# Moving and regrouping the weight loads, maxima and splits beside the attention stage

## The chip, the cores and the metric

The kernel runs on one core of a Trainium2 chip. The metric is device time in microseconds; the median of three runs is given. The core has five instruction streams: TensorE (matmuls and transposes, PE), VectorE (DVE), ScalarE (ACT), GpSimd (POOL) and SyncE (SP, which here only issues DMAs). Each stream runs in order and waits on semaphores.

## The reference

```
attn: q, k, v [4, 8, 576, 64]; scores = q k^T / 8
      heads 0..3: keep 0 <= i - j < 32        (local)
      heads 4..7: keep j <= i, i = j mod 32   (strided)
      softmax, times v  -> x [2304, 512]
moe:  h = x @ w_in [512, 2048];  g = h * sigmoid(1.702 h);  x2 = g @ w_out [2048, 512]
moe2: logits = x2 @ w_gate + log1p(exp(x2 @ w_noise)) * noise;  top 2 of 8 experts, softmax of the two
      out += weight * (relu(x2 @ w1[e]) @ w2[e])        for the two experts e of each token
```

## The kernel before, in words

The kernel has three stages. The first is attention: the 8 heads of 4 batches are taken two at a time, as 16 pairs numbered 0 to 15. Pairs 0 and 1 of each batch are local, 2 and 3 strided. The second stage is the dense feed-forward layer on groups of 256 tokens, the third the routed experts. The change touches the first stage alone.

Every float32 matmul of the feed-forward layers is done as three float16 matmuls. A weight matrix w is scaled by a power of two and split into hi = fp16(w) and lo = fp16(w - hi). The scale needs the largest absolute value of the matrix. So for `w_in` the order is: load raw words into `stage_raw` (L466), take the maximum of each part on VectorE (`w_in_max`, L1076), combine the parts, spread the result over the partitions with one matmul into `ps_all` (L1793, semaphore all_max), reduce it (L1204, semaphore all_read), work out scale and inverse in five dependent tiny instructions (`power_of_two`, L1081 to L1086), then write hi on ScalarE (`weights_hi`, L854) and lo on VectorE (`weights_lo`, L1139). `w_out` is then loaded into the same `stage_raw`, part by part as the lo of `w_in` frees it (L472), and its maxima are taken before attention ends. The first two groups of attention output x get the same treatment: `group_max` (L1115), `group_hi` (L836), `group_lo` (L1111). All this is done beside attention, in slots fixed by hand: the tables `MAX_IN`, `PARTS_IN`, `MAX_OUT`, `HI_X`, `LO_X` say at which pair i each part is taken.

The attention rounds are a software pipeline written out by hand. In round i, TensorE turns q of pair i+2 (L1608 where local, L1616 where strided), finishes p times v of pair i-1 (L1697 local, L1710 strided), turns k of pair i+2, writes masks, turns the probabilities p of pair i (L1677), does the scores of pair i+2 (L1663) and the first half of p times v of pair i. ScalarE evacuates q and k (L810), keeps the finished output (`keep_out`, L831), takes the exponentials of pair i+1 (`exps`, L824) and evacuates p in two pieces (L818), with a `weights_hi` after each piece where one is due. VectorE, in its iteration i, does `weights(i)` (the maxima and splits due there), then `sums(i+1)` (row sums L1104, reciprocal L1107), then `max_and_sub(i+2)` (L1095, L1097). GpSimd multiplies by the reciprocals (`norm`, L653) and TensorE can turn p of a pair only after that.

In iterations 3, 7 and 11 (after pairs 2, 6 and 10) VectorE first waits for `ps_all` and for the output of the pair before to be kept, reduces it and works out the factors, before anything else of the iteration. In the same rounds TensorE waits for all_read before the first half of p times v, because `ps_all` lies in the bank that this writes.

At the end, round 14 runs four pieces of the first feed-forward matmuls ahead (`mlp_ahead`, L1739, 48 matmuls), then spreads the maximum of `w_out` (L1803), which VectorE reduces (L1175), and round 15 closes the stage.

SyncE issues every load of this stage on one queue: q and k of a pair are four DMAs of 144 KB (L458 local, L462 strided), v is 432 KB in three DMAs or 288 KB in two (L395, L399, L405). Before the loop it issues q and k of pairs 0 to 3, v of 0 and 1, the gate weights, and eighths 0, 1 and 2 of `w_in`, 512 KB each. Step i of its loop waits until k of pair i+2 is turned, issues q and k of pair i+4, waits for the turning of p of pair i (p_turned), issues v of pair i+3, waits for the second piece, and issues eighth i+3 of `w_in` or the eighths of `w_out` that `W_OUT_AT` names.

## Time and profile before

| | |
|---|---|
| median of three runs (976.17 to 979.78) | 976.63 us |
| profiled execution, its own time | 979.78 us |
| its span, first to last instruction | 978.1 us |
| PE busy in the span | 930.0 us (95%) |
| DVE busy | 564.3 us (58%) |
| ACT busy | 303.1 us (31%) |
| mean granted TensorE clock | 0.972 |
| chain that ended last, by engine | PE 45%, DVE 33%, ACT 10%, DMA 5% |

The profile is of the slowest of the three runs. Its own time holds 1.7 us outside the span. The granted clock is given as a share of 2.4 GHz: 1.00 is 2.4 GHz, 0.50 is 1.2 GHz. "Idle before" names what ended an idle time of an engine. A duration of an instruction and the step from its start to the next start can differ by some tenths of a microsecond, because neighbours overlap; sums along an engine go by starts.

### The profile page before, as it was taken

How to read it: one execution, taken by the hardware profiler on the slowest of the kernel's cores; microseconds unless marked ns; L12 is line 12 of the kernel's file. 1: busy time of each engine (PE TensorE's matmuls, PEld its weight loads, DVE VectorE, ACT ScalarE, POOL GpSimd, SP SyncE). 2: the span in 40 equal slices, each digit the busy share in tenths (PEclk: the TensorE clock that was granted, in tenths of full speed). 3: DMA queues.
4: the chain of work that ended last, by engine and by line, in shares of the span. 5: the costliest groups of instructions: out<-in, count | busy, mean ns of one | idle time of the engine just before them, and what ended most of it. 6: DMA issues, size and time to landing. Idle time of an engine off the chain costs nothing.

```text
span 978.1 us, 25171 instructions
## 1 busy us (share of the span) xinstructions
PE 930.0 (95%) x10467; PEld 665.2 (68%) x10468; DVE 564.3 (58%) x1030; ACT 303.1 (31%) x412; POOL 198.2 (20%) x269
## 2 busy tenths in 40 slices
PE   8999899999999999999999799899999999999992
PEld 5787686757667675756657576567767777777771
DVE  3469958888888888889986543232332332332231
ACT  4469662423333342334313131111111111111110
POOL 5112200000000000000251332233323333333321
PEclk9689899999999999999999999999999999999997
DMA  9979619675756566575567348565665758474340
GB/s 211 220 172 227 154 40 334 219 264 199 266 187 219 189 215 236 183 256 193 186 225 235 77 114 226 188 189 154 168 185 155 197 131 224 115 222 123 79 87 23
DMA packets 138853, 178.18 MB, mean 182 GB/s; under 512 B 88407, under 2 KB 100695, under 8 KB 136736
## 3 DMA queue, kind: packets, MB, share of 16 engines
q1 hardware_dynamic: 81440, 138.14, 45.2%
q0 software_dynamic: 9600, 27.69, 9.4%
q10 hardware_dynamic: 47744, 11.35, 6.9%
q8 instruction: 53, 0.87, 0.4%
q14 instruction: 16, 0.13, 0.0%
HBM read 112.09 MB, written 53.55 MB: 169 GB/s over the span
## 4 chain that ended last, share of the span: by engine, by line
PE 45%; DVE 33%; ACT 10%; DMA 5%; issue 3%; SPq 1%; POOLq 0%; POOL 0%; ACTq 0%; DVEq 0%
PE bank L1947 19%; PE bank L1956 17%; DVE sc L1076 8%; DVE arena L1265 7%; ACT arena L902 5%; DVE arena L1220 4%; DMA arena<-out,arena 2%; DVE arena L1218 2%; DMA out<-arena 2%; PE bank L1608 2%; PE bank L1847 1%; PE bank L1677 1%; ACT arena L848 1%; DVE x L1111 1%; DVE w_out_s L1139 1%
## 5 line engine op out<-in xcount | busy, mean ns | idle before, releaser
L1739 PE MATMUL bank<-x,w_in_s 128*128 128x256 f16 (+1 forms) x1728 | 195.4, 274 | 0.0
L1847 PE MATMUL bank<-w_out_s,arena 128*128 128x512 f16 x864 | 192.2, 379 | 3.0 <-DVE arena L1220 2.9
L1739 PEld LDWEIGHTS bank<-x,w_in_s 128*128 128x128 f16 x1728 | 169.4, 98 | 23.9
L1847 PEld LDWEIGHTS bank<-w_out_s,arena 128*128 128x128 f16 x864 | 82.7, 98 | 100.0 <-DVE arena L1220 6.4
L1538 DVE TENSOR_TENSOR arena<-arena 128x512 f32<-128x512 f32 x37 | 25.6, 692 | 168.6 <-ACT arena L999 92.8
L1947 PEld LDWEIGHTS bank<-arena,w_out_s 128*128 128x128 f16 x2016 | 114.5, 98 | 5.8 <-issue 0.7
L1947 PE MATMUL bank<-arena,w_out_s 128*128 128x128 f16 x2016 | 116.9, 219 | 0.6 <-issue 0.6
L1947 PEld LDWEIGHTS bank<-arena,w_in_s 128*128 128x128 f16 x1920 | 109.1, 98 | 6.7 <-issue 2.2
L1947 PE MATMUL bank<-arena,w_in_s 128*128 128x128 f16 x1920 | 111.6, 219 | 1.5 <-DMA arena<-arena 1.4
L1956 PE MATMUL bank<-w_out_s,arena 128*128 128x512 f16 x480 | 108.6, 383 | 4.4 <-DVE arena L1533 4.4
L1956 PE MATMUL bank<-w_in_s,arena 128*128 128x512 f16 x480 | 106.9, 379 | 2.3 <-DVE arena L1533 2.3
L1076 DVE TENSOR_REDUCE sc<-arena 128x1 f32<-128x512 f32 (+2 forms) x50 | 102.2, 2045 | 3.7 <-ACT arena L908 3.4
L1531 DVE CAST arena<-arena 128x512 f16<-128x512 f32 x82 | 35.3, 431 | 116.7 <-ACT arena L994 102.6
L994 ACT ACTIVATE arena<-bank 128x512 f32<-128x512 f32 x82 | 49.0, 597 | 169.6 <-PE bank L1947 150.7
L1265 DVE SCALAR_TENSOR_TENSOR arena<-arena,sc 128x4096 f16<-128x4096 f32 x16 | 71.7, 4482 | 26.4 <-ACT arena L902 26.4
L1956 PEld LDWEIGHTS bank<-w_out_s,arena 128*128 128x128 f16 x480 | 46.5, 99 | 57.7 <-issue 6.9
L902 ACT ACTIVATE arena<-arena,sc 128x4096 f16<-128x4096 f32 x16 | 59.3, 3709 | 82.9 <-DVE sc L1086 82.9
L999 ACT ACTIVATE arena<-bank,arena 128x512 f32<-128x512 f32 x40 | 27.5, 687 | 183.6 <-PE bank L1956 180.4
L1956 PEld LDWEIGHTS bank<-w_in_s,arena 128*128 128x128 f16 x480 | 46.1, 98 | 54.5 <-DVE arena L1533 2.1
L717 POOL DMA_INDIRECT arena<-out,arena x37 | 43.5, 1177 | 131.8 <-DMA out<-arena 116.6
L722 POOL DMA_INDIRECT out<-arena x40 | 41.7, 1043 | 107.1 <-DVE arena L1538 101.4
L1533 DVE TENSOR_TENSOR arena<-arena 128x512 f16<-128x512 f32 x82 | 56.8, 693 | 2.8
(219 smaller groups left out, 830.8 us busy)
## 6 DMA issues: line engine op xcount, KB each, us to landing
arena<-in_moe_w SPq DMA_DIRECT2D x16, 2048.0 KB, 9.7
split_weights<-arena SPq DMA_DIRECT2D x16, 2048.0 KB, 7.4
w_in_s<-split_weights SPq DMA_DIRECT2D x32, 512.0 KB
w_out_s<-split_weights SPq DMA_DIRECT2D x32, 512.0 KB
arena<-in_q SPq DMA_DIRECT2D x32, 144.0 KB, 3.2
arena<-in_k SPq DMA_DIRECT2D x32, 144.0 KB, 3.9
out<-zeros SPq DMA_DIRECT2D x1, 4608.0 KB, 21.5
x_rows<-arena SPq DMA_DIRECT2D x18, 256.0 KB, 2.2
```

Of the source, the lines that this page charges most:

```text
L717: pool.indirect_dma_start(out=prior[b4 % 2], out_offset=None, in_=out, in_offset=bass.IndirectOffsetOnAxis(ap=cur[b4], axis=0), bounds_che ...
L722: pool.indirect_dma_start(out=out, out_offset=bass.IndirectOffsetOnAxis(ap=cur[b4], axis=0), in_=ysb[b4 % 2], in_offset=None, bounds_check ...
L902: nc.scalar.activation(halves[:, 0], raw[m], ACT.Copy, scale=col(S_U + m)).then_inc(S["unit_hi"], 1)
L994: nc.scalar.activation(hf[half], ps_dh[half], ACT.Relu, scale=DOWN).then_inc(S["relu_done"], 1)
L1076: return nc.vector.tensor_reduce(dst, src, AX.X, ALU.max, apply_absolute_value=True)
L1220: nc.vector.scalar_tensor_tensor(lo, gf[fq % 2], of_group(G_X, t), hi, ALU.mult, ALU.subtract).then_inc(S["g_lo"], 1)
L1265: nc.vector.scalar_tensor_tensor(halves[:, 1], raw[m], col(S_U + m), halves[:, 0], ALU.mult, ALU.subtract).then_inc(S["unit_lo"], 1)
L1533: V.tensor_tensor(lo, hf[half], hi, ALU.subtract).then_inc(S["h_lo"], 1)
L1739: last = mm(dst, w_in_s[:, w_part, c, f * P:(f + 1) * P], group_half(x_part, t)[:, c], start=(c == 0 and w_part + x_part == 0), stop=(c == ...
L1847: last = mm(ps_x[j], g[par][:, g_part, f, j * P:(j + 1) * P], w_out_s[:, w_part, f], start=(n == 0), stop=(n == 3 * FC - 1))
L1947: last = mm(ps_dh[half][:, n * P:(n + 1) * P], w1_of(w_par, w_part, c, f), xt[par][:, x_part * DC + c], start=(c == 0 and w_part + x_part ...
L1956: last = mm(ps_y[par], h[par][:, h_part, f * P:(f + 1) * P], w2_of(w_par, w_part, f), start=(n == 0), stop=(n == 3 * EFC - 1))
```

## The change

Loads and maxima of `w_in` and loads of `w_out` go from eight parts of 512 KB to four quarters of 1 MB. Before the loop only quarter 0 of `w_in` is loaded, where eighths 0, 1 and 2 were; quarters 1, 2 and 3 follow in the loop steps of pairs 4, 5 and 7 (`W_IN_AT`, i = 2, 3, 5 in the new numbering, which is two ahead of the old). The quarters of `w_out` go out in the loop steps of pairs 13 and 14 and twice after the loop. The loop's waits for p_turned are gone. The splits are still done by eighths. The tables of iterations change: maxima of `w_in` in iterations 2 to 5, group maxima both in 8, hi of `w_in` in rounds 8 to 12 instead of 7 to 11 and lo one later, maxima of `w_out` in 12 to 14 instead of 9 and 12 to 14, hi of group 1 in round 13 instead of 14, lo of group 1 in iteration 14 instead of 15. In iterations 3, 7 and 11 VectorE now does the weights and the row sums first, then reduces `ps_all`, then does `max_and_sub`, and works out the factors last.

```diff
--- before.py
+++ after.py
@@ -67,14 +67,12 @@
 
 QUARTERS = 4
 BUSY = 16
-SPLIT_OUT = 15
+MAX_IN, SPLIT_OUT = 2, 15
 LAST_IN, LAST_X, LAST_OUT = 6, 10, 14
-MAX_X = 7
-MAX_IN = {2: (0, 1), 3: (2,), 4: (3, 4), 5: (5, 6), 6: (7,)}
-PARTS_IN = {7: (0,), 8: (1, 2), 9: (3, 4), 10: (5, 6), 11: (7,)}
-HI_X, LO_X = {12: 0, 14: 1}, {13: 0, 15: 1}
-MAX_OUT = {9: (0,), 12: (1, 2), 13: (3, 4), 14: (5, 6, 7)}
-assert max(MAX_IN) <= LAST_IN < min(PARTS_IN)
+MAX_X = 8
+PARTS_IN = {8: (0, 1), 9: (2, 3), 10: (4,), 11: (5, 6), 12: (7,)}
+MAX_OUT = {12: (0, 1), 13: (2, 3, 4), 14: (5, 6, 7)}
+assert MAX_IN + QUARTERS <= LAST_IN < min(PARTS_IN) - 1
 CONSTS = 12 + 2 + 1 + 4 + 1 + SQ // SRES + 2
 
 FULL = (2 * TOK) // P
@@ -300,7 +298,7 @@
 
 
         S = {n: sem(n) for n in (
-            "consts_pool busy_set qk_in0 qk_in1 v_in0 v_in1 v_in2 v_in3 w_raw0 w_raw1 w_raw2 w_raw3 w_raw4 w_raw5 w_raw6 w_raw7 "
+            "consts_pool busy_set qk_in0 qk_in1 v_in0 v_in1 v_in2 v_in3 w_raw0 w_raw1 w_raw2 w_raw3 "
             "small_in noise_in t_done t_evac s_done mx_done sub_done exp_done sum_done rr_done norm_done pv_done "
             "o_kept x_hi x_lo x_max x_all x_step x_scaled raw_max scaled step split_hi split_lo "
             "raw_in0 raw_in1 unit_max unit_all unit_scaled unit_hi unit_lo unit_out "
@@ -312,7 +310,7 @@
             "held turning out_zero zero_done prior_in0 prior_in1 y_sum y_out w_even w_odd xg_zero"
         ).split()}
         qk_in = [S["qk_in0"], S["qk_in1"]]
-        w_raw = [S[f"w_raw{i}"] for i in range(2 * QUARTERS)]
+        w_raw = [S[f"w_raw{i}"] for i in range(QUARTERS)]
         v_in = [S[f"v_in{i}"] for i in range(4)]
         raw_in = [S["raw_in0"], S["raw_in1"]]
         x2_store = [S["x2_store0"], S["x2_store1"]]
@@ -447,6 +445,8 @@
 
         @block.sync
         def _(sp):
+            w_in_raw = stage_raw.rearrange("p (c f) -> p c f", c=DC)
+            w_out_raw = stage_raw.rearrange("p (c n) -> p c n", c=FC)
 
             def load_qk(b, hp):
                 par = hp % 2
@@ -463,19 +463,19 @@
                                          ).then_inc(qk_in[par], 16)
 
             def load_w_in(n):
-                sp.dma_start(eighth_raw(n), w_in.rearrange("(c p) (a f) -> p c a f", p=P, a=2)[:, n // 2, n % 2]
+                c = DC // QUARTERS
+                sp.dma_start(w_in_raw[:, n * c:(n + 1) * c], w_in.rearrange("(c p) f -> p c f", p=P)[:, n * c:(n + 1) * c]
                              ).then_inc(w_raw[n], 16)
 
             def load_w_out(n):
-                c = FC // QUARTERS // 2
-                sp.wait_ge(S["split_lo"], n + 1)
-                sp.dma_start(eighth_raw(n).rearrange("p (c n) -> p c n", c=c),
+                c = FC // QUARTERS
+                sp.wait_ge(S["split_lo"], 2 * n + 2)
+                sp.dma_start(w_out_raw[:, n * c:(n + 1) * c],
                              w_out.rearrange("(c p) n -> p c n", p=P)[:, n * c:(n + 1) * c]).then_inc(w_raw[n], 16)
 
             load_qk(0, 0)
             load_qk(0, 1)
             load_w_in(0)
-            load_w_in(1)
             sp.wait_ge(S["t_done"], 4)
             load_qk(0, 2)
             load_v(sp, 0, 0)
@@ -484,27 +484,25 @@
             load_v(sp, 0, 1)
             sp.dma_start(wg[:, :, 0:E], w_gate.rearrange("(c p) e -> p c e", p=P)).then_inc(S["small_in"], 16)
             sp.dma_start(wg[:, :, E:16], w_noise.rearrange("(c p) e -> p c e", p=P)).then_inc(S["small_in"], 16)
-            load_w_in(2)
-
-            W_OUT_AT = {8: (0,), 9: (1, 2), 10: (3, 4), 11: (5, 6)}
-            for i in range(NPAIR - PAIRS):
-                q_turned, p_turned = 8 * i + 12, 8 * i + 14
-                sp.wait_ge(S["t_done"], q_turned)
-                load_qk((i + 4) // PAIRS, (i + 4) % PAIRS)
-                if i == 0:
+
+            W_IN_AT, W_OUT_AT = {2: 1, 3: 2, 5: 3}, {11: 0, 12: 1}
+            for i in range(2, NPAIR - 2):
+
+                sp.wait_ge(S["t_done"], 8 * i - 4)
+                load_qk((i + 2) // PAIRS, (i + 2) % PAIRS)
+                if i == 2:
                     load_v(sp, 0, 2)
-                sp.wait_ge(S["t_done"], p_turned)
-                if i > 0:
-                    sp.wait_ge(S["pv_done"], i)
-                load_v(sp, (i + 3) // PAIRS, (i + 3) % PAIRS)
-                sp.wait_ge(S["t_done"], p_turned + 2)
-                if i + 3 < 2 * QUARTERS:
-                    load_w_in(i + 3)
-                for n in W_OUT_AT.get(i, ()):
-                    load_w_out(n)
+                else:
+                    sp.wait_ge(S["pv_done"], i - 2)
+                load_v(sp, (i + 1) // PAIRS, (i + 1) % PAIRS)
+                if i in W_IN_AT:
+                    load_w_in(W_IN_AT[i])
+                if i in W_OUT_AT:
+                    load_w_out(W_OUT_AT[i])
             sp.wait_ge(S["pv_done"], NPAIR - PAIRS)
             load_v(sp, BATCH - 1, PAIRS - 1)
-            load_w_out(2 * QUARTERS - 1)
+            load_w_out(2)
+            load_w_out(3)
 
             sp.dma_start(noise_sb[:], noise.rearrange("(t p) e -> p t e", p=P)).then_inc(S["noise_in"], 16)
 
@@ -873,8 +871,8 @@
                     exps(i + 1)
                 evac_pt(p_use, hp, 0)
                 parts = PARTS_IN.get(i, ())
-                if HI_X.get(i) == 0:
-                    group_hi(0)
+                if i in (LAST_X + 2, LAST_X + 3):
+                    group_hi(i - LAST_X - 2)
                 elif parts:
                     weights_hi(parts[0], w_in_s, S_WI, 1)
                     parts = parts[1:]
@@ -885,7 +883,6 @@
                     weights_hi(n, w_in_s, S_WI, 1)
                 if i == NPAIR - 2:
                     exps(i + 1)
-                    group_hi(1)
                 if i == NPAIR - 1:
                     act.wait_ge(S["scaled"], 3)
                     gelu(0, 0)
@@ -1121,13 +1118,13 @@
             def w_in_max(n):
 
                 dve.wait_ge(w_raw[n], 16)
-                step(absmax(col(PART_MAX + n), eighth_raw(n)))
-                if n == 2 * QUARTERS - 1:
-                    absmax(col(B_MAX), col(PART_MAX, 2 * QUARTERS)).then_inc(S["raw_max"], 1)
+                step(absmax(col(PART_MAX + n), quarter_raw(n)))
+                if n == QUARTERS - 1:
+                    absmax(col(B_MAX), col(PART_MAX, QUARTERS)).then_inc(S["raw_max"], 1)
 
             def w_out_max(n):
 
-                dve.wait_ge(w_raw[n], 32)
+                dve.wait_ge(w_raw[n // 2], 32)
                 step(absmax(col(PART_MAX + n), eighth_raw(n)))
                 if n == 2 * QUARTERS - 1:
                     absmax(col(B_MAX), col(PART_MAX, 2 * QUARTERS)).then_inc(S["raw_max"], 1)
@@ -1157,19 +1154,19 @@
                     dve.wait_ge(S["small_in"], 32)
                     nc.vector.tensor_reduce(col(B_MAX), wg[:], AX.XY, ALU.max, apply_absolute_value=True
                                             ).then_inc(S["raw_max"], 1)
-                for n in MAX_IN.get(i, ()):
-                    w_in_max(n)
-                if i in (MAX_X, MAX_X + 1):
+                if MAX_IN <= i < MAX_IN + QUARTERS:
+                    w_in_max(i - MAX_IN)
+                if i == MAX_X:
                     dve.wait_ge(S["o_kept"], PAIRS + 1)
-                    step(group_max(PART_MAX + i - MAX_X, i - MAX_X))
-                if i == MAX_X + 1:
+                    step(group_max(PART_MAX, 0))
+                    step(group_max(PART_MAX + 1, 1))
                     absmax(col(B_MAX), col(PART_MAX, 2)).then_inc(S["raw_max"], 1)
                 for n in PARTS_IN.get(i - 1, ()):
                     weights_lo(n, w_in_s, S_WI, 0)
                 for n in MAX_OUT.get(i, ()):
                     w_out_max(n)
-                if i in LO_X:
-                    group_lo(LO_X[i])
+                if i in (LAST_X + 3, LAST_X + 4):
+                    group_lo(i - LAST_X - 3)
                 if i == NPAIR - 1:
                     dve.wait_ge(S["all_max"], 4)
                     nc.vector.tensor_reduce(col(WO_ALL), ps_all_out, AX.X, ALU.max).then_inc(S["out_max"], 1)
@@ -1198,17 +1195,18 @@
                 w_out_lo(i)
 
             for i in range(NPAIR):
+                weights(i)
+                if i + 1 < NPAIR:
+                    sums(i + 1)
                 if i - 1 in ALL_OF:
                     dve.wait_ge(S["all_max"], i // PAIRS + 1)
                     dve.wait_ge(S["o_kept"], i + 1)
                     nc.vector.tensor_reduce(col(ALL_OF[i - 1]), ps_all, AX.X, ALU.max).then_inc(S["all_read"], 1)
+                if i + 2 < NPAIR:
+                    max_and_sub(i + 2)
+                if i - 1 in ALL_OF:
                     dve.wait_ge(S["all_read"], i // PAIRS + 1)
                     weights_factors(i - 1)
-                weights(i)
-                if i + 1 < NPAIR:
-                    sums(i + 1)
-                if i + 2 < NPAIR:
-                    max_and_sub(i + 2)
             weights_factors(NPAIR - 1)
 
             def split_g(t, par, fq):
```

## Rows read from the trace of the kernel before

**Rows 1.** Stretches of the span: engine busy us (instructions), PEclk, DMA share, GB/s.

```profile
0.00:128.70 128.70, 115.62 (x2740) 92.39 (x2741) 85.82 (x115) 74.25 (x165) 35.72 (x64) 0.85 0.80 187
...
29.61:56.92 27.31, 27.31 (x539) 23.03 (x534) 14.00 (x17) 12.42 (x29) 3.71 (x3) 0.50 0.90 203
...
63.40:69.60 6.20, 6.16 (x206) 5.16 (x205) 3.79 (x7) 3.85 (x10) 1.28 (x2) 1.00 0.81 181
```

**Rows 2.** Waits of TensorE, 0 to 135 us: total us, times, longest.

```profile
PE bank L1677 <- POOL arena L653: 4.7, 4, 1.9
```

**Rows 3.** TensorE in time: start, us, line, [idle before]: rounds 1 to 3, round 5.

```profile
26.99 0.69 PE L1697 MATMUL bank<-arena 96*64 96x64 f32 x16
...
29.30 0.19 PE L1623 MATMUL bank<-busy_in 128*128 128x28 bf16 x1 [1.63 <-DMA arena<-in_k]
...
39.75 1.53 PE L1608 MATMUL bank<-ident,arena 48*64 48x48 f32 x48
...
57.81 0.71 PE L1616 MATMUL bank<-ident,arena 96*128 96x96 f32 x6
```

**Rows 4.** SyncE in time: the load of eighth 2 of w_in.

```profile
20.30 0.51 SPq L466 DMA_DIRECT2D arena<-in_moe_w_in  x1
```

**Rows 5.** DMAs by line, k of pair 4, then pair 5: first and last start, landing.

```profile
L458 SPq DMA_DIRECT2D arena<-in_k x2: 432/818/1204, 21.8 to 23.1; - x2
...
DMA to landing us min/median/max: 4.4/4.8/6.1
...
L458 SPq DMA_DIRECT2D arena<-in_k x2: 433/1043/1653, 26.7 to 28.4; - x2
...
DMA to landing us min/median/max: 7.1/7.7/8.2
```

**Rows 6.** Round 7 in time: ScalarE, VectorE (up to iteration 8), TensorE.

```profile
72.99 1.01 ACT L824 ACTIVATE arena<-arena 128x960 f32<-128x960 f32 x1
...
72.07 0.29 DVE L1204 TENSOR_REDUCE sc<-bank 128x1 f32<-128x128 f32 x1 [1.36 <-ACT x L831]
...
73.53 1.22 DVE L1115 TENSOR_REDUCE sc<-x 128x1 f32<-128x1024 f32 x1
...
80.82 1.15 DVE L1104 TENSOR_REDUCE arena<-arena 128x10 f32<-128x960 f32 x1
...
75.12 0.67 PE L1710 MATMUL bank<-arena 36*64 36x36 f32 x32
```

**Rows 7.** Rounds 11 to 14 in time: ScalarE exps(12), then VectorE.

```profile
97.40 1.01 ACT L824 ACTIVATE arena<-arena 128x960 f32<-128x960 f32 x1
...
96.47 0.29 DVE L1204 TENSOR_REDUCE sc<-bank 128x1 f32<-128x128 f32 x1 [0.95 <-ACT x L831]
...
98.29 2.47 DVE L1139 SCALAR_TENSOR_TENSOR w_in_s<-arena,sc,w_in_s 128x1024 f16<-128x1024 f32 x2
...
100.68 1.15 DVE L1104 TENSOR_REDUCE arena<-arena 128x10 f32<-128x960 f32 x1
...
101.99 1.10 DVE L1095 TENSOR_REDUCE arena<-bank 128x10 f32<-128x960 f32 x1
...
104.20 1.27 DVE L1139 SCALAR_TENSOR_TENSOR w_in_s<-arena,sc,w_in_s 128x1024 f16<-128x1024 f32 x1
...
105.39 2.47 DVE L1076 TENSOR_REDUCE sc<-arena 128x1 f32<-128x1024 f32 x2
...
107.89 1.16 DVE L1104 TENSOR_REDUCE arena<-arena 128x10 f32<-128x960 f32 x1
...
110.62 2.46 DVE L1076 TENSOR_REDUCE sc<-arena 128x1 f32<-128x1024 f32 x2
...
113.12 1.28 DVE L1111 SCALAR_TENSOR_TENSOR x<-x,sc 128x1024 f16<-128x1024 f32 x1
...
114.32 0.75 DVE L1104 TENSOR_REDUCE arena<-arena 128x16 f32<-128x576 f32 x1
...
116.67 3.72 DVE L1076 TENSOR_REDUCE sc<-arena 128x1 f32<-128x1024 f32 x3
```


## The prediction

> **What bounds the kernel now.** I read the table of stretches first. The change touches only attention and what runs beside it, and that stage ends at about 128.7 us [rows 1]. What follows has the same instructions before and after, in the same order, and starts from what the stage leaves; so I carry a shift of the stage's end to the end of the kernel one to one. In the stage VectorE is busy 85.8 of 128.7 us and TensorE's mean granted clock is 0.85 [rows 1]; neither alone says what binds, so I read it in time, stretch by stretch.
>
> First stretch, to about 57 us: transfers and the clock. TensorE ends the first half of p times v of pair 1 at 27.7 and stands still until q and k of pair 4 are there; its next matmul is at 29.30, and the row names in_k for 1.63 us of idle time [rows 3]. The last k DMA of that pair is issued at 23.1 and lands 6.1 us later, at 29.2 [rows 5]. Right behind this idle time the granted clock is 0.50 (1.2 GHz) for 27.3 us, with the DMA engines busy 90% of it at 203 GB/s [rows 1]. Rounds 3 and 4 run in that stretch and take 57.81 - 39.75 = 18.1 us [rows 3], where a round at 1.00 takes 6.2 us [rows 1]. Next stretch, from 63 us: rounds of 5.7 to 6.5 us, passed between TensorE, ScalarE and VectorE. Last stretch, rounds 11 to 15: VectorE. It works nearly without a gap from 96.47 on [rows 7], and what TensorE waits for is the normalized p: 4.7 us in four waits [rows 2], each behind VectorE's row sums.
>
> The terms are worked out against the profiled execution, 979.78 us (span 978.1 and 1.7 around it). It is the slowest of three; the median is 3.15 us lower. I add the change to the median, since nothing here makes it depend on what differs between these runs, except the length of the slow-clock stretch, which stays in the range.
>
> **The early loads.** Eighth 2 of w_in, 512 KB, is issued at 20.30 [rows 4], just ahead of q and k of pair 4 on the same queue. The change takes it from there. At the 203 GB/s of that stretch 512 KB are 2.6 us, so k of pair 4 lands at 29.2 - 2.6 = 26.6 instead, before the 27.7 at which TensorE asks. The wait of 1.63 us goes. What is late next: by the time of q and k of pair 5, both versions have put the same bytes into the queue (2 MB of w_in, the same q, k and v), because quarter 1 now goes out in the first loop step. That k lands at 28.4 + 8.2 = 36.6 before [rows 5], behind a queue that never ran dry, and I keep 36.6 for after. Before, TensorE asked for it only at 39.75, since round 2 ran at the slow clock. Now round 2 can start at 27.7 at the full clock, is done 6.2 us later at 33.9, and TensorE stands still for 2.7 us until 36.6. That is longer than the idle time that preceded the fall before, so I expect the clock to fall there, and rounds 3 and 4 to run slowly as they did. Gain: 39.75 - 36.6 = 3.2 us at the start of round 3. Least: if the clock falls at 29.6 all the same, round 2 runs as before, 1.6 us early, and 1.6 us stay; none stays if larger loads ahead of pair 6 make that one late. Most: full clock throughout; then each round is bounded by its transfers. To the start of round 5, three rounds of 6.2 us from 27.7 plus 2.7 of waiting end at 49.0, plus 2.6 for the extra 512 KB that then lie ahead of pair 6: 51.6 against 57.81, 6.2 us. I take 3.2, range 0 to 6.2.
>
> The Trainium skill (TensorE: Matmul & The Clock Gate, Terms) prices time at the low clock at that time times one minus the granted share. By that the 27.3 us cost 13.7 us, and keeping the clock would give 13.7 instead of 6.2. The rows say less, since part of those rounds waits for transfers anyhow.
>
> The dropped waits for p_turned on SyncE let v and w_in go out one or two microseconds sooner, behind q and k of the same step; nothing on TensorE waits for v in these rows. I cost it at nothing, and at up to 1 us if a megabyte lies in front of q and k of pair 6; that is inside the bound of 0. The maxima of w_in cost VectorE the same words in four instructions as in eight, saving four fixed starts of under 0.1 us each beside idle time: nothing. Quarter 3 must be there in iteration 5; it is issued with round 3's k and has a round and a half.
>
> **Iterations 7 to 9.** Before, VectorE waits 1.36 us for the kept output and reduces ps_all at 72.07 [rows 6]. After, the row sums of pair 8 come first. They need exps(8), which end at 72.99 + 1.01 = 74.0. Then 74.0 + 1.31 (row sums and reciprocal of a local pair, 100.68 to 101.99 [rows 7]) + 0.33 (the reduce) = 75.6, when TensorE may start p times v of pair 7, which it starts at 75.12 before: 0.5 us late. The hi part that leaves ScalarE in this round gives up to 1.0 us, but it is behind this wait and is lost. VectorE goes on: + 2.21 (max_and_sub, local, 101.99 to 104.20) + 1.15 (factors) + 2.5 (both group maxima, one of them 1.22 [rows 6]) = 81.5 for the row sums of pair 9, against 80.82: 0.7 us late, of the same delay. I take +0.6 us, bounds -1.0 (ScalarE's gain comes through) and +1.0. In iterations 9 and 10 VectorE has less to do than before, but the rounds are then passed on by ScalarE, still with two hi parts in rounds 8 and 9, and by TensorE: its free time is not turned into anything.
>
> **Iterations 11 to 14, the main loss.** With that 0.6, exps(12) end at 98.4 + 0.6 = 99.0 [rows 7]. VectorE is free by about 96.7 and idles until then. From there it is the bound, and its work up to the row sums of pair 14 is, by steps from start to start [rows 7]: row sums 12, 1.31; reduce and factors, 1.82 (96.47 to 98.29); max_and_sub 13, 2.21; lo of eighths 5 and 6, 2.39 (98.29 to 100.68); maxima 0 and 1 of w_out, 2.50 (105.39 to 107.89); row sums 13 and max_and_sub 14, 2.73 (107.89 to 110.62); lo of 7, 1.19 (104.20 to 105.39); three maxima, 3.72; lo of group 0, 1.20 (113.12 to 114.32). Sum 19.1, so 99.0 + 19.1 = 118.1 against 114.32: 3.8 us late. Before, the same span held one maximum less and did one lo and one maximum in the light iterations 8 and 9. The norm of pair 14, TensorE's turning of it, and the four pieces of mlp_ahead follow it directly, so the stage ends 3.8 us later, this time the 0.6 included. The three maxima of iteration 14 and the lo of group 1, now ahead of row sums 15, lie beside mlp_ahead, which covers them: they end at about 127, it at 132. Without that cover they would cost 1.2 us.
>
> Gains inside: the wait of 1.55 us at round 12 for norm(12) goes, since the row sums of pair 12 start at 99.0 and not at 100.68; it returns in round 13 and 14 as a longer one. Bounds of this term: 2.0 (the light rounds 9 to 11 run 1.8 us faster than I allow) and 5.5 (mlp_ahead, which runs at 0.50 for most of its time before, meets a longer slow stretch, 1.7 us more).
>
> **Sum.** -3.2 + 3.8 = +0.6 us: 980.4 for the profiled execution, 977.2 for the median.
>
> **Rivals.**
> A, forecast: early gain of about 3, late loss of about 4, 976 to 979.
> B, the clock falls as before. For it: rounds with the small transposes leave little work per microsecond even when TensorE is occupied. Gain 1.6, loss 3.8: +2.2, 978.8.
> C, full clock through rounds 2 to 4. For it: the wait that preceded the fall is gone. Against: transfers still bind and TensorE must stand still before round 3 and 4. -6.2 + 3.8 = -2.4, 974.2; with the late loss at its lower bound 2.0, 972.4, and with ScalarE's 1.0 as well, 971.4.
> D, slower: the pile on VectorE. Row sums of pairs 13 and 14 come behind 4.9 and 6.1 us of weight work in iterations 12 and 13 instead of 3.7 and 3.7. It decides from the point where the early gain is under 1 us: either the clock falls at 29.6, or 1 MB ahead of pair 6 starves round 4 and the slow clock lasts into round 6. Then 0 + 5.5 = +5.5: 982.1.
> E, the loads don't matter and the early stretch is unchanged because another transfer (v, or the slowest of the DMA engines) holds k of pair 4 up to 29: 0 + 3.8, 980.4; it is B with nothing gained.
>
> **Chances.** A 0.40, B and E 0.22, C 0.15, D 0.23. A measurement here tells a change from none at about 0.5%, 4.9 us: faster means under 971.7, slower over 981.5. Under 971.7 lies the far end of C and some of what I have not seen: 0.09. Over 981.5 lie D, mostly, and a little of E: 0.26. The rest, 0.65, is the same. A's own range is 975 to 979; the range for 8 in 10 goes from 971.5 (C at its bounds) to 983.5 (D with another microsecond of waiting).
>
> **What would show it.** Right: no idle time of TensorE named in_k near 28 us, but one of 2 to 3 us near 34 to 36; the clock 1.00 in round 2, then 0.50; round 3 starting near 36.6 and round 5 near 54.6; TensorE's wait for norm(12) gone and those for norm(13) and norm(14) longer, 3 us or more each; VectorE without a gap from the row sums of pair 12 on; L1175 near 129 (128.4 before, +0.6). Wrong: the clock at 1.00 through to round 5 (C), or 0.50 past 60 us (D); row sums of pair 14 less than 2 us after or more than 6 us after those before, measured from the end of exps(12); or a shift of the stages behind 128.7 us that isn't that of the stage's end.

## The result and the profile after

The changed kernel takes 983.98 us, the median of seven runs (982.05 to 989.32), against 978.11 for the kernel before in seven runs beside it (976.08 to 981.26). The ratio is 1.007, with a 95% interval of 1.004 to 1.010: slower, by about 5.9 us, where 977.2 and a range of 971.5 to 983.5 were forecast. The forecast started from 976.63, the median of three runs; the kernel before is at 978.11 in the seven. So 1.5 us of the miss of 6.8 lie in that, and 5.3 in the change itself: +5.9 measured for +0.6 forecast.

The profiled execution of the changed kernel is its fastest, and not one of the seven: 979.09 us, span 977.4. That is less than the 979.78 of the profiled execution before, so the two totals say nothing; the stages have to be read one by one. The end of the attention stage is where VectorE reduces the last `ps_all`: L1175 before, L1172 after. That row starts at 128.38 before and 133.99 after, 5.6 us later. How near this is to the 5.9 us between the medians is partly luck: a second profile of the changed kernel has the row at 136.10. The row before:

```profile
128.38 0.29 DVE L1175 TENSOR_REDUCE sc<-bank 128x1 f32<-128x128 f32 x1 [5.74 <-PE bank L1803]
```

**Behind the stage.** From there to about 610 us the same matmul of the second and third stages starts 5.6 us later in the trace after, wherever one compares: matmul number 2800 from the start at 132.77 and 138.38, number 5100 at 448.76 and 454.36, number 6500 at 604.83 and 610.45. What turns the totals round is one event in the kernel before that the trace after lacks. First a row of TensorE there (start, length, idle time ahead of it), then the piece of the chain of waits that leads to it:

```profile
623.00 3.52 PE L1956 MATMUL bank<-w_out_s,arena 128*128 128x512 f16 x9 [4.40 <-DVE arena L1533]
...
611.70 8.95 DMA arena<-out,arena
```

A DMA of 9 us leaves TensorE idle for 4.4 us, and a stretch at the low clock follows; together about 6.2 us. Such an event (a DMA of 6.9 to 9.7 us between 605 and 634 us, and 2.9 to 5.5 us of idle TensorE behind it) shows in 6 of the 14 profiles of this study, of kernels of both kinds. In the other eight the work behind the stage takes 843 to 846 us, in these six 847 to 854. So in these traces a shift of the stage does carry on one to one, and a total of one execution can't be read against another. How often the event falls into the timed runs of each kernel is not known, since only profiled executions show it.

**The early loads.** The wait for k of pair 4 [rows 3] is gone. Its last DMA is issued at 21.6 and takes at most 4.3 us, so it is there by 26 us, where [rows 5] have it at 29.2:

```profile
L458 SPq DMA_DIRECT2D arena<-in_k x2: 431/436/441, 21.1 to 21.6; - x2
...
DMA to landing us min/median/max: 3.0/3.0/4.3
```

TensorE goes into round 2 at 28.54 without a wait, at full clock, which it keeps until 32.2. And it gets hardly further than before. TensorE in time, after (start, length, line, idle time ahead):

```profile
28.65 0.91 PE L1606 MATMUL bank<-ident,arena 48*64 48x48 f32 x48
29.50 0.42 PE L1695 MATMUL bank<-arena 96*64 96x32 f32 x7
33.18 1.22 PE L1695 MATMUL bank<-arena 96*64 96x32 f32 x17 [3.26 <-issue]
...
40.70 0.92 PE L1606 MATMUL bank<-ident,arena 48*64 48x48 f32 x48
...
42.53 0.49 PE L1606 MATMUL bank<-ident,arena 48*64 48x48 f32 x17
44.31 0.68 PE L1606 MATMUL bank<-ident,arena 48*64 48x48 f32 x31 [1.29 <-issue]
...
54.48 0.68 PE L1695 MATMUL bank<-arena 96*64 96x64 f32 x14
56.36 0.33 PE L1695 MATMUL bank<-arena 96*64 96x64 f32 x2 [1.20 <-issue]
57.12 0.71 PE L1614 MATMUL bank<-ident,arena 96*128 96x96 f32 x6 [0.42 <-issue]
```

TensorE stops three times in the middle of a run of like matmuls, after 7 of 24, after 17 of 48 and after 14 of 16, and each time for nothing that the profile shows ("issue"). These stops and the short one at 57.12 are 6.2 us in sum. Round 3 starts at 40.70 (39.75 before), round 5 at 57.12 (57.81). Of the two queues in the DMA view of 28 to 35 us, one carries instructions, the other the loads:

```profile
q1 hardware_dynamic: 1871, 1.61, 107.9%
q8 instruction: 2, 0.03, 2.5%
...
arena<-in_moe_w_in SPq DMA_DIRECT2D x1, 1024.0 KB, 10.3
```

In 28 to 35 us 16-KB packets of instructions go through the same DMA engines as a 1-MB load that takes 10.3 us to land. One of them is under way from 30.5 to 31.8, and TensorE resumes at 33.18; others end at 42.8 and 54.8, and TensorE resumes at 44.31 and 56.36. Every profile but that of the kernel before has such stops, 40 in all: each comes after 594, 718, 843 or 1092 matmuls of the trace, and each ends 1.0 to 1.7 us after a packet of that queue has ended. (In 9 of them a further stop of 0.3 to 0.4 us, as the one at 57.12, comes two matmuls after the last.) So what TensorE lacks there are its own instructions.

**The late part.** VectorE, rounds 11 to 15, and the end of the stage; it answers to [rows 7], where the row sums of pairs 12, 13 and 14 stand at 100.68, 107.89 and 114.32:

```profile
91.81 0.75 DVE L1101 TENSOR_REDUCE arena<-arena 128x16 f32<-128x576 f32 x1 [0.41 <-ACT arena L822]
...
98.50 1.15 DVE L1101 TENSOR_REDUCE arena<-arena 128x10 f32<-128x960 f32 x1 [2.23 <-ACT arena L822]
...
104.06 2.48 DVE L1136 SCALAR_TENSOR_TENSOR w_in_s<-arena,sc,w_in_s 128x1024 f16<-128x1024 f32 x2
106.45 2.47 DVE L1073 TENSOR_REDUCE sc<-arena 128x1 f32<-128x1024 f32 x2
108.95 1.15 DVE L1101 TENSOR_REDUCE arena<-arena 128x10 f32<-128x960 f32 x1
...
111.68 1.63 DVE L1136 SCALAR_TENSOR_TENSOR w_in_s<-arena,sc,w_in_s 128x1024 f16<-128x1024 f32 x1
113.23 3.71 DVE L1073 TENSOR_REDUCE sc<-arena 128x1 f32<-128x1024 f32 x3
116.98 1.28 DVE L1108 SCALAR_TENSOR_TENSOR x<-x,sc 128x1024 f16<-128x1024 f32 x1
118.18 0.74 DVE L1101 TENSOR_REDUCE arena<-arena 128x16 f32<-128x576 f32 x1
...
133.99 0.29 DVE L1172 TENSOR_REDUCE sc<-bank 128x1 f32<-128x128 f32 x1 [7.39 <-PE bank L1801]
```

From the row sums of pair 11 to those of pair 14 it is 26.37 us, where the same took 22.04 before: 4.3 us more. The row sums of pair 11 before:

```profile
92.28 0.75 DVE L1104 TENSOR_REDUCE arena<-arena 128x16 f32<-128x576 f32 x1
```

Ahead of the row sums of pair 14 lie 6.5 us of splits and maxima (111.68 to 118.18), the pile of what follows. Then ScalarE and TensorE in the same rounds, after:

```profile
112.85 0.76 ACT L816 ACTIVATE arena<-bank 96x384 f32<-96x384 f32 x2 [0.38 <-PE bank L1675]
118.37 1.15 ACT L834 ACTIVATE x<-x,sc 128x1024 f16<-128x1024 f32 x1 [4.75 <-DVE x L1108]
119.42 0.74 ACT L816 ACTIVATE arena<-bank 96x384 f32<-96x384 f32 x2
```

```profile
114.38 0.69 PE L1695 MATMUL bank<-arena 96*64 96x64 f32 x16
119.94 1.55 PE L1695 MATMUL bank<-arena 96*64 96x32 f32 x24 [4.88 <-ACT arena L816]
121.42 2.28 PE L1675 MATMUL bank<-ident,arena 128*128 128x128 f32 x8
```

The hi part of group 1 (L834), moved to round 13, waits 4.75 us on ScalarE for the lo part of group 0 (L1108), which VectorE does behind its three maxima. Behind L834 in ScalarE's order is the second copy of the turned p(13) (L816), and for that TensorE idles 4.88 us. In this stretch, 111.1 to 121.4, TensorE is busy 4.24 of 10.30 us at a mean granted clock of 0.81; it is at 1.2 GHz from 117.6 to 131.2:

```profile
111.10:121.40 10.30, 4.24 (x115) 3.66 (x115) 10.13 (x11) 3.24 (x6) 2.28 (x2) 0.81 0.47 111
```

### The profile page after: what moved, and what is told of

The parts are those of the page before. It is cut to its first block, busy times and chain, and to the rows that moved or that the text cites. A ratio compares the mean times of both kernels' runs of the same rounds, so it can differ in the third digit from the quotient of the medians.

```text
span 977.4 us, 25136 instructions
## 1 busy us (share of the span) xinstructions
PE 925.3 (95%) x10467; PEld 661.2 (68%) x10468; DVE 564.0 (58%) x1026; ACT 302.6 (31%) x412; POOL 196.4 (20%) x269
## 4 chain that ended last, share of the span: by engine, by line
PE 48%; DVE 34%; ACT 9%; issue 4%; DMA 2%; POOL 0%; ACTq 0%; POOLq 0%; SPq 0%; DVEq 0%
PE bank L1945 20%; PE bank L1954 19%; DVE sc L1073 8%; DVE arena L1263 7%; ACT arena L899 5%; DVE arena L1218 4%; DVE arena L1216 2%; PE bank L1675 2%; PE bank L1606 1%; PE bank L1845 1%; PE bank L1661 1%; ACT arena L846 1%; DVE x L1108 1%; DVE w_out_s L1136 1%; PE bank L1695 1%
## 5 line engine op out<-in xcount | busy, mean ns | idle before, releaser
L1073 DVE TENSOR_REDUCE sc<-arena 128x1 f32<-128x512 f32 (+3 forms) x46 | 101.6, 2209 | 3.6 <-ACT arena L905 3.4
```

The lines of the kernel that those rows point to most:

```text
L1073: return nc.vector.tensor_reduce(dst, src, AX.X, ALU.max, apply_absolute_value=True)
```

## The experiments

Each ran beside the kernel before on the same chip. To read the cause I use three stretches of the first stage in each one's profiled execution: to the row sums of pair 5, from there to those of pair 11, and from there to the end of the stage. The ratio comes from all timed runs of both kernels and can differ by 0.2% from the ratio of the two medians; "stops" is the sum of TensorE's idle time put down to "issue" between 16 and 64 us.

```
                        to p.5  5 to 11  11 to 14  11 to end  end     stops  ratio [95%]
before                   54.68   37.60    22.04     36.10    128.38   0.0
after                    53.48   38.33    26.37     42.18    133.99   6.2    1.007  [1.004, 1.010]
change, once more        55.90   38.03    26.37     42.17    136.10   7.7    1.010  [1.006, 1.014]
group 1 back             54.83   38.02    26.03     40.14    132.99   4.9    1.007  [1.003, 1.011]
factors first            53.74   46.57    25.38     40.55    140.86   9.4    1.005  [1.002, 1.009]
eighth loads back        50.64   37.15    26.03     40.47    128.26   3.2    1.001  [0.998, 1.004]
w_in later               48.62   38.25    27.04     42.34    129.21   1.5    0.998  [0.995, 1.002]
three maxima left out    54.19   45.72    22.28     38.02    137.93   11.3   1.000  [0.998, 1.003]
late part spread         53.72   39.97    24.13     37.57    131.26   7.6    1.000  [0.997, 1.003]
quarter loads only       53.26   38.94    22.01     36.96    129.16   6.9    0.999  [0.996, 1.003]
quarter loads, again     54.99   37.27    22.03     33.62    125.88   5.6    1.000  [0.997, 1.004]
before, loads later      48.82   39.46    22.03     33.62    121.90   3.7    1.000  [0.997, 1.003]
before, later, again     48.84   38.70    22.04     35.97    123.51   4.0    1.001  [0.997, 1.004]
spread and later         47.20   43.41    23.72     37.26    127.87   2.7    1.002  [0.999, 1.004]
```

The stretches are of one execution each, and three kernels were profiled twice. From pair 11 to 14 the two profiles of a kernel agree within 0.02 us, to the end they do not: 36.96 and 33.62, 33.62 and 35.97, though 42.18 and 42.17 for the change. The piece behind the row sums of pair 14 goes with the granted clock: 11.6 us at 0.92, 13.4 to 14.4 at 0.63 to 0.76, 15.0 to 15.8 at 0.59 to 0.67. And the profiled execution is the fastest of its kernel in after, the change once more, eighth loads back and the first of loads later, the slowest in factors first, three maxima left out, and spread and later. So the end of the stage in one row can't be held against the ratio beside it.

**Group 1 back.** Of the changed kernel, hi of group 1 goes back to round 14 and lo to iteration 15.

```diff
-                if i in (LAST_X + 2, LAST_X + 3):
-                    group_hi(i - LAST_X - 2)
+                if i == LAST_X + 2:
+                    group_hi(0)
...
                 if i == NPAIR - 2:
                     exps(i + 1)
+                    group_hi(1)
...
-                if i in (LAST_X + 3, LAST_X + 4):
-                    group_lo(i - LAST_X - 3)
+                if i in (LAST_X + 3, LAST_X + 5):
+                    group_lo((i - LAST_X - 3) // 2)
```

> The changed kernel with hi and lo of group 1 put back where they were before (round 14 and iteration 15). Theory P (pile on VectorE, and beside it a wait of ScalarE): in the changed kernel ScalarE stands 4.75 us in round 13, because hi of group 1 waits for lo of group 0, and the second piece of p of pair 13 lies behind it; TensorE stands 4.88 us. Without it that piece goes out near 115, but the row sums of pair 14 still start near 118, so p of pair 14 is turned near 120.5 instead of 121.4, and the stage ends 1 to 3 us earlier (L1172 near 131 to 133 instead of 134.0): 981 to 983 for the median. Rival W (the wait of ScalarE is the whole loss): L1172 near 129, median 978 to 979. Rival E (the early loads are the loss): no difference to the changed kernel, 984.

Measured: 985.82 us (980.62 to 994.88), 1.007; the expected 981 to 983 were missed. In the trace the idle time of 4.88 us is gone and TensorE waits 2.21 us for the normalized p instead:

```profile
116.59 2.40 PE L1696 MATMUL bank<-arena 96*64 96x64 f32 x40
121.20 2.28 PE L1676 MATMUL bank<-ident,arena 128*128 128x128 f32 x8 [2.21 <-POOL arena L651]
```

From pair 11 to the end it is 2.0 us less than after: 0.3 up to the row sums of pair 14, 0.9 from there to the turning of its p (2.32 us for 3.24), and 0.8 behind it, where the clock was higher. The wait of L834 is real, but at most 0.9 us can be put down to it, and not safely: with three maxima left out (below) it is 1.0 us long, and TensorE, then at 1.2 GHz, takes up p of pair 14 3.23 us behind the row sums all the same. It is not the main cause: the row sums of pair 14 stay late, and the median does not fall.

**Eighth loads back.** The changed kernel with the loads and maxima of `w_in` by eighths, and the loop of SyncE with its waits for p_turned, as before; the rest is the change's.

```diff
-MAX_IN, SPLIT_OUT = 2, 15
+SPLIT_OUT = 15
+MAX_IN = {2: (0, 1), 3: (2,), 4: (3, 4), 5: (5, 6), 6: (7,)}
...
+                sp.wait_ge(S["t_done"], p_turned + 2)
+                if i + 3 < 2 * QUARTERS:
+                    load_w_in(i + 3)
```

> The changed kernel with w_in loaded and its maxima taken by eighths at the places of before, and the loop waits of SyncE as before; all the rest of the change stays. Theory P: TensorE's three stops inside a run of matmuls (3.26, 1.29 and 1.20 us, waiting for nothing that the profile shows) go, the wait for k of pair 4 and the slow clock from 30 to 57 us come back, round 5 starts near 57.8; the late part is as in the changed kernel, row sums of pair 14 near 119, end near 134.5; median 983 to 985. Rival E: the early loads are the loss: median near 978.

Measured: 980.62 us, 1.001; 983 to 985 were expected, with the clock low from 30 to 57 us and round 5 near 57.8, and all three were missed. The wait for k is back, 1.90 us; the stops for "issue" are 3.2 us, about half of those after; pair 5 comes at 50.64. The pile stays (26.03). So with the pile in place, the old loads are worth about 5 us by the medians: 1.0 us over the kernel before beside it, where the change is 5.9 over.

**Quarter loads only**, run twice: the kernel before with `w_in` in four loads of 1 MB at the change's steps.

```diff
-MAX_IN = {2: (0, 1), 3: (2,), 4: (3, 4), 5: (5, 6), 6: (7,)}
+MAX_IN = {2: (0,), 3: (1,), 4: (2,), 5: (3,)}
...
+            W_IN_AT = {0: 1, 1: 2, 3: 3}
...
-                if i + 3 < 2 * QUARTERS:
-                    load_w_in(i + 3)
+                if i in W_IN_AT:
+                    load_w_in(W_IN_AT[i])
```

> The kernel before with the early part alone: w_in loaded in four quarters of 1 MB at the steps of the change, maxima in iterations 2 to 5; everything else as before. Theory P: k of pair 4 is there in time, TensorE stops inside matmul runs appear as in the changed kernel, round 5 starts at 57 +- 1, row sums of pair 14 near 113.5 to 114.5, L1175 near 128; median within 1.5 us of before, 977 to 979. Rival E: median 983 or more.

> The kernel of e3 (before, with the early part of the change alone) in five rounds. If the early part of the change neither gains nor loses, because the wait for k has only become stops for instructions: within 1.5 us of before. If the megabyte loads cost in themselves: 2 to 4 us over before. If my forecast of the early part was right after all: 3 us under before.

Measured: 977.26 and 973.89 us, 0.999 and 1.000. The medians are 2.3 us under those of the kernel before beside them both times, but the ratio over all runs is within 0.1% of 1, and its interval reaches 0.36% to either side. Alone, the large loads neither gain the forecast 3 us nor cost anything that can be told from the spread, though TensorE's stops are 6.9 and 5.6 us in sum.

**Factors first.** The changed kernel with the old order in iterations 3, 7 and 11: the reduction of `ps_all` and the factors ahead of the row sums.

```diff
             for i in range(NPAIR):
-                weights(i)
-                if i + 1 < NPAIR:
-                    sums(i + 1)
                 if i - 1 in ALL_OF:
...
+                    dve.wait_ge(S["all_read"], i // PAIRS + 1)
+                    weights_factors(i - 1)
+                weights(i)
+                if i + 1 < NPAIR:
+                    sums(i + 1)
```

> The changed kernel with the reduction of the spread maximum and the factors put back to the front of iterations 3, 7 and 11. Theory P: iteration 11 again waits for the kept output and does 1.8 us of factors before lo of eighth 4 and the row sums of pair 12, which start near 99.5 to 100 instead of 98.5; the work after it is the same less 1.8, so row sums of pair 14 come near 117.5 to 118.2, as in the changed kernel or up to 0.7 us earlier; median 983 to 984.5. Rival O (the new order is what costs): 980 or less.

Measured: 984.00 us, 1.005, not told from the change. So the order of the factors shows no part in the loss.

**w_in later.** The changed kernel with quarters 1 to 3 loaded from round 5 on. The four maxima of `w_in` are then all taken of quarter 0, so its factor is another number.

```diff
-            W_IN_AT, W_OUT_AT = {2: 1, 3: 2, 5: 3}, {11: 0, 12: 1}
+            W_IN_AT, W_OUT_AT = {7: 1, 8: 2, 9: 3}, {11: 0, 12: 1}
...
+                if scaled == 1 and n % 2 == 0:
+                    act.wait_ge(w_raw[n // 2], 16)
...
-                dve.wait_ge(w_raw[n], 16)
-                step(absmax(col(PART_MAX + n), quarter_raw(n)))
+                dve.wait_ge(w_raw[0], 16)
+                step(absmax(col(PART_MAX + n), quarter_raw(0)))
```

> The changed kernel with quarters 1 to 3 of w_in loaded from round 5 on instead of rounds 0 to 3, so that 3 MB fewer compete in the first 50 us; the maximum is taken four times of quarter 0 (this part of the computation is changed). Theory F (instructions of TensorE come late because the DMA engines are full): the stops inside runs of matmuls (3.3, 1.3, 1.2 us in the changed kernel) shrink to under 0.5 us in all, there is no wait for k, the clock stays at 1.00 past 35 us, round 5 starts at 47 to 51 instead of 57, and the median is 5 to 9 us under the changed kernel: 975 to 979. Rival G (they come late by themselves, whatever the traffic): the stops stay at 4 us or more in all and the median is within 2 us of 984.

Measured: 976.13 us (971.09 to 979.44), 0.998. TensorE's rows, the same stretch as the rows of the early loads above:

```profile
29.03 0.42 PE L1697 MATMUL bank<-arena 96*64 96x32 f32 x7
29.60 0.74 PE L1697 MATMUL bank<-arena 96*64 96x32 f32 x17 [0.15 <-issue]
...
34.11 0.32 PE L1710 MATMUL bank<-arena 36*64 36x36 f32 x7
34.63 0.59 PE L1710 MATMUL bank<-arena 36*64 36x36 f32 x25 [0.20 <-issue]
...
37.11 0.69 PE L1608 MATMUL bank<-ident,arena 48*64 48x48 f32 x17
38.94 1.10 PE L1608 MATMUL bank<-ident,arena 48*64 48x48 f32 x31 [1.14 <-issue]
...
50.53 0.71 PE L1616 MATMUL bank<-ident,arena 96*128 96x96 f32 x6 [0.23 <-ACT arena L816]
```

The stop after 7 of 24 falls from 3.26 to 0.15 us, and round 5 starts at 50.53 instead of 57.12. The DMA engines move less; the stretch 20 to 50 us, after and here:

```profile
20.00:50.00 30.00, 25.02 (x643) 20.51 (x643) 16.17 (x20) 15.10 (x37) 5.90 (x4) 0.83 0.90 213
```

```profile
20.00:50.00 30.00, 27.73 (x772) 22.68 (x771) 20.28 (x24) 18.29 (x45) 5.90 (x4) 0.89 0.74 168
```

So with 3 MB moved away the stops shrink from 6.2 to 1.5 us, where under 0.5 was expected. Between the first two stops 124 matmuls run and between the next two 125, each with a weight load of its own: about 250 instructions, in every kernel at the same places of the code.

The amount of traffic alone doesn't order the profiles, though. In the same 30 us the five with `w_in` by eighths move 217 to 226 GB/s and stop for 0.0 to 4.0 us in sum; the eight with 1-MB loads at the change's steps move 200 to 218 GB/s and stop for 4.9 to 11.3. Spread and later has the most traffic of all:

```profile
20.00:50.00 30.00, 26.29 (x763) 21.39 (x750) 18.52 (x26) 17.89 (x45) 7.22 (x5) 0.94 0.98 226
```

That points at the size of a load that lies ahead; but the steps at which the loads go out differ too, and no run changes the size alone.

**Three maxima left out.** The changed kernel without the maxima of eighths 2 to 4 of `w_out`; its factor comes from eighths 5 to 7 alone.

```diff
-MAX_OUT = {12: (0, 1), 13: (2, 3, 4), 14: (5, 6, 7)}
+MAX_OUT = {12: (0, 1), 14: (5, 6, 7)}
```

> The changed kernel without the three maxima of w_out in iteration 13 (left out of the computation, with those of iteration 12 out of the combination). Theory P (pile on VectorE): lo of group 0 and the row sums of pair 14 come 3.7 us earlier, near 114.5, ScalarE's wait in round 13 falls from 4.75 to about 1 us, the stage ends 3.5 to 5 us earlier (L1172 near 129 to 130.5); median 979 to 981. Rival W2 (the loss is in the order of the waits, the pile has slack): less than 1.5 us earlier.

Measured: 979.43 us, 1.000. Pair 11 to pair 14 falls from 26.37 to 22.28 us, and ScalarE's wait with it to 1.0 us. VectorE, iterations 13 and 14:

```profile
119.44 1.63 DVE L1136 SCALAR_TENSOR_TENSOR w_in_s<-arena,sc,w_in_s 128x1024 f16<-128x1024 f32 x1
120.99 1.27 DVE L1108 SCALAR_TENSOR_TENSOR x<-x,sc 128x1024 f16<-128x1024 f32 x1
122.19 0.74 DVE L1101 TENSOR_REDUCE arena<-arena 128x16 f32<-128x576 f32 x1
```

3.7 us of VectorE work taken away from one place give back 4.1 us there and 4.2 us by the time of the stage's end (38.02 for 42.18). The profiled execution ends its stage late all the same, at 137.93 where 129 to 130.5 was expected, since its early stops happened to be 11.3 us and its clock low from 60 to 70 us; it is the slowest of its ten, and the median does not show that.

**Late part spread.** Nothing left out: the changed kernel with group 1 back, the group maxima in iterations 7 and 8, and the maxima of `w_out` from iteration 11.

```diff
-MAX_X = 8
+MAX_X = 7
-MAX_OUT = {12: (0, 1), 13: (2, 3, 4), 14: (5, 6, 7)}
+MAX_OUT = {11: (0, 1), 12: (2,), 13: (3, 4), 14: (5, 6, 7)}
...
```

> The changed kernel with group 1 back in round 14 and iteration 15, the group maxima one each in iterations 7 and 8, and the maxima of w_out 0 and 1 in iteration 11 (where VectorE idles 2.2 us), 2 in 12, 3 and 4 in 13. Theory P: VectorE's work between the exponentials of pair 12 and the row sums of pair 14 falls by 2.5 us, these come near 115.7, and the stage's end (L1173) is 3.5 to 5 us earlier than the changed kernel's 134.0; median 979 to 981. Rival: under 1.5 us.

Measured: 977.99 us, 1.000. From pair 11 to pair 14 it is 24.13 us instead of 26.37, the 2.2 us that were forecast as 2.5; to the end 37.57 instead of 42.18.

**Before, loads later**, run twice: the kernel before with eighths 2 to 6 of `w_in` loaded one or two loop steps later, so that none but 0 and 1 goes out ahead of the loop.

```diff
-            load_w_in(2)
+            W_IN_AT = {1: (2,), 2: (3,), 3: (4, 5), 4: (6, 7)}
-MAX_IN = {2: (0, 1), 3: (2,), 4: (3, 4), 5: (5, 6), 6: (7,)}
+MAX_IN = {2: (0, 1), 4: (2,), 5: (3, 4), 6: (5, 6, 7)}
...
```

> The kernel before with the eighths of w_in later: none in loop step 0, eighth 2 in step 1, 3 in step 2, 4 and 5 in step 3, 6 and 7 in step 4, maxima 2; 3, 4; 5, 6, 7 in iterations 4, 5, 6. 1 MB fewer lies ahead of q and k of pairs 4 to 7. Theory F: no wait for k of pair 4, shorter stops, round 5 starts at 51 to 54 instead of 57.8; two heavy iterations cost 1 to 2 us; median 2 to 5 us under before. Rival G: within 1.5 us of before.

> The kernel of e7 (before, with the eighths of w_in later) in five rounds, for the question whether it beats before. Theory F: 2 to 5 us under before; its stops of TensorE under 4 us in all. Rival G: within 1.5 us of before.

Measured: 977.05 and 977.46 us, 1.000 and 1.001. No wait for k, stops of 3.7 and 4.0 us, pair 5 at 48.8 in both. Yet the ratio does not move, and the expected 2 to 5 us under the kernel before were missed both times. In the two traces the stage ends 5 to 6.5 us before that of the kernel before; that this shows in no ratio is not explained.

**Spread and later**: both edits on the changed kernel, the late part spread and the loads by eighths, later.

> The changed kernel with both repairs: the late part spread as in e8 (group 1 back, group maxima in 7 and 8, maxima of w_out 0, 1 in iteration 11, 2 in 12, 3 and 4 in 13) and w_in by eighths at the later steps of e7. If late pile and early traffic are the two causes and add: 4 us from the first, 3 to 5 from the second against the changed kernel, so 975 to 977, 1 to 3 us under before. If only the late pile counts: 978 to 980.

Measured: 977.97 us, 1.002; the expected 975 to 977 were missed. Pair 5 comes at 47.20, the earliest of all, but the next stretch is 43.41 us, with a low clock from 66 to 79.7 us. **The change, once more**, to have its size twice:

> The changed kernel once more, unchanged, beside the three that follow, to size the loss on one chip and to see the early stops a second time. From the row sums of pair 11 to those of pair 14: 26.4 +- 0.5 us as in its first profile (22.0 before); the early stops of TensorE 5 us or more in all; median 5 to 7 us over before.

Measured: 986.59 us (980.70 to 987.46, six runs), 1.010, 10.5 us over the kernel before where 5 to 7 were expected, and the wait of 4.88 us on TensorE again. No version here beats the kernel before.

## Why the prediction was wrong

**Late part: right in place, too small, and its one good figure is luck.** The row sums of pair 14 were forecast at 118.1 and started at 118.18. But the 118.1 leaves out the early gain; with the 3.2 us of the sum it would be 114.9. Counted from the row sums of pair 5, which lie ahead of all that the late part moves, the row sums of pair 14 come 64.70 us behind, for 59.64 before: 5.1 us more, where 3.8 were forecast. Of that, 0.7 us lie before pair 11 (0.6 forecast), exps(12) came about 0.5 us later after pair 11, and pair 12 to pair 14 took 19.68 us, 3.8 more than from the end of exps(12) before, for 19.1 and 3.2 forecast. TensorE's wait at round 12 for the normalized p is gone, and those at rounds 13 and 14 are longer, as forecast (2.45 us, and the 4.88 us that hides the other). The rows for pair 5, before and after:

```profile
54.68 1.15 DVE L1104 TENSOR_REDUCE arena<-arena 128x10 f32<-128x960 f32 x1 [2.10 <-ACT arena L824]
```

```profile
53.48 1.15 DVE L1101 TENSOR_REDUCE arena<-arena 128x10 f32<-128x960 f32 x1 [0.68 <-ACT arena L822]
```

Taking three maxima out of the pile, or spreading it, brings the ratio from 1.007 and 1.010 to 1.000. But so do the two runs that keep the pile and change when and how `w_in` is loaded (1.001 and 0.998, with 26.03 and 27.04 us from pair 11 to pair 14). So as far as the ratios go the pile is needed for the loss, and so are the large early loads; neither is its cause alone.

**The end of the stage: one wait was missed.** "The norm of pair 14, TensorE's turning of it, and the four pieces of mlp_ahead follow it directly, so the stage ends 3.8 us later." I moved hi of group 1 to round 13 without asking for what it waits: lo of group 0, which I had put behind the maxima in the very same sum, and p(13) is queued behind it on ScalarE. TensorE so takes up p(14) at 121.42 instead of 116.64 (4.8 us later, where the row sums are 3.9 later) and runs the rest at the low clock: the 48 matmuls of mlp_ahead take 8.01 us for 7.59. From the row sums of pair 14 to the end it is 15.8 us for 14.1, 1.7 us more, 0.9 of it at p(14) and the rest behind it. After, then before:

```profile
125.89 8.01 PE L1737 MATMUL bank<-x,w_in_s 128*128 128x256 f16 x48
```

```profile
116.64 0.66 PE L1677 MATMUL bank<-ident,arena 128*128 128x128 f32 x4 [1.94 <-POOL arena L653]
...
120.70 7.59 PE L1739 MATMUL bank<-x,w_in_s 128*128 128x256 f16 x48
```

How much of the 1.7 us is the wait and how much the clock isn't separated: this piece took 15.7 us also where the wait was only 1.0 us (three maxima left out), and 14.1 with group 1 back.

**Early loads: the failed step.** "Now round 2 can start at 27.7 at the full clock, is done 6.2 us later at 33.9 ... Gain: 39.75 - 36.6 = 3.2 us at the start of round 3." Round 2 did start at 28.54 at the full clock. But TensorE then ran dry of instructions, for 6.2 us in sum, which no row of the kernel before had as a wait. There, all of rounds 2 to 4 ran at 1.2 GHz [rows 1], the packets of instructions came too, and TensorE never stopped for one; that the slower pace hid them is my reading. Round 3 started 0.95 us later than before instead of 3.2 earlier, and round 5 0.7 us earlier instead of 3.2. The idle time of 2 to 3 us for k of pair 5 that I named did not show; k was there. In all eight profiles with loads by quarters at the change's steps pair 5 comes at 53.3 to 55.9 us, the 54.68 of before in their midst. At the row sums of pair 5 the gain is 1.2 us in this trace, and in the ratios of quarter loads only (0.999 and 1.000) it is nothing that can be told. At rounds 3 and 5 this is rival D's condition, an early gain under 1 us, by a mechanism that I had not named. Its price of 5.5 us lies near the 5.9 measured by luck: it had 1.7 us for a longer slow stretch in mlp_ahead, which took 0.4 us more, and it had nothing for the missed wait. The four starts of maxima that I priced at under 0.1 us each were 0.6 us in sum (2.28 us for a quarter, 1.21 for an eighth); they lie beside idle time all the same.

The Trainium skill (Runtime: NRT & Kernel Launch, Instruction fetch mechanics) says that an engine's instructions are fetched through a DMA queue of its own in blocks of 16 KiB, or 256 instructions, and that this is mostly hidden. The 16-KB packets and the stops some 250 instructions apart agree with the first; that it is hidden does not hold here, with up to 5.5 us in one stop. The Trainium skill (DMA: Bandwidth & Descriptors, Queues, rings and completion order) has each DMA engine take turns between queues packet by packet; no run here shows the turns themselves.

**Iterations 7 to 9** were right in size: forecast 0.6 us later; the row sums of pair 8 start 1.5 us earlier than before and those of pair 9 0.3 later, and from pair 5 to pair 11 it is 0.7 us more (38.33 for 37.60). The second profile of the change has 0.4.

**The sum, by the traces.** To the row sums of pair 5 -1.2 us, where -3.2 were forecast at round 3; from there to the end of the stage +0.7 and +6.1, where 3.8 were forecast for both. Together +5.6. So the early term is off by 2.0 us and the late one by 3.0, both to the same side. The carry was right: behind the stage these two traces stay 5.6 us apart up to 610 us.

**What stays open.** The two halves don't add up. Large loads cost nothing that shows on the kernel before (0.999, 1.000), and neither does the late pile with the loads by eighths (1.001); only together are they 0.7 to 1.0% slower. In the profiles one sees half of it: with the old loads in the changed kernel pair 5 comes at 50.64, 2.6 to 5.3 us ahead of the quarters, which pays for the pile. But then the kernel before should gain as much over its version with quarters, and it does not. The waits for p_turned were put back only together with the eighth loads, so their part isn't separated either. Nor is it shown what makes the instruction packets late: the run that moved loads away changed the amount of traffic, the rates over all profiles speak for the size of a load, and the steps were never held fixed. And the event of 6 us behind the stage may fall into the timed runs of one kernel more often than into those of another; no run rules that out as a part of the 0.7%.

Where the low clock falls varies too. It was 0.50 for 27 us in the one profile of before; with the same loads in the changed kernel it was not.

## What to carry to other kernels

When an instruction is moved, write down what it waits for in its new place and what is queued behind it on its engine; a wait of 4.75 us came here from a part that was itself moved at no cost. A wait that is taken away where the DMA engines are 90% busy can come back under another name, here 1.63 us for k as 6.2 us for instructions. So ask what the next transfer, be it the engine's own instructions, allows. And sum the work of the busiest engine between two events on the path: that gave 19.1 us here for 19.7 measured.

## What the hardware showed that was not expected

TensorE stands still for its own instructions, 0.2 to 5.5 us at a time, always at the same places of the code, and it resumes 1.0 to 1.7 us after a 16-KB packet of the instruction queue has ended. It does so when the DMA engines are near full: 1.5 us in sum with 168 GB/s in the stretch from 20 to 50 us, 6.2 with 213 GB/s; but only 2.7 with 226 GB/s where the loads are of 512 KB. A stretch at 1.2 GHz follows such stops at no fixed place (32.2 to 39.1 and 45.9 to 49.3 us after; 66 to 79.7 in the run of both edits). And a DMA in the third stage takes 7 to 10 us in some executions, whatever the kernel, and the work behind the first stage is then 847 to 854 us instead of 843 to 846. It is one reason why a single profile of each version would here have said "no change".
